# Sparse attention on one core: the inverse row sums are turned in 32 by 32 blocks and brought to the transposed sums by DMA, so that these are transposed once and not twice

## The reference

```python
# 1: attention over 8 global keys and a window of 96, with a slope per head
scores = q @ k.T / 8 + bias;  scores[~keep] = -1e9
a = exp(scores - max);  a = a / (sum(a) + 1e-9);  x = a @ v          # x: (2, 768, 512)
# 2: token mix of rank 32 and a feed-forward part
u = x + (x.T @ U @ V).T;  x = u + relu(u @ w_ch1) @ w_ch2            # 512 -> 2048 -> 512
# 3: gated part
h = relu(x @ w_in);  a, b = split(h);  out = (a * (w_spatial @ norm(b) + b_spatial)) @ w_out
```

## Time and profile before

| | |
|---|---|
| median of three runs | 494.84 us |
| span of the profiled execution, first to last instruction | 493.2 us |
| what lies around the span, against the median | 1.6 us |
| PE busy | 489.0 us (99%) |
| DVE, ACT, POOL busy | 310.2, 222.0, 250.2 us |
| the 24 steps, from `turn(0)` to `hidden(0)` | 9.24 to 92.15 us |
| granted TensorE clock over the span | 1.00 |

### The profile page before, as it was taken

The page is one execution under the profiler, slowest core; times in us unless marked ns, Lnnn a source line. Parts: engine busy times, 40 slices in busy tenths (PEclk is TensorE's granted clock), DMA queues, the critical chain, the costliest instruction groups (busy, mean ns, idle before and its releaser), DMA issues.

```text
span 493.2 us, 7961 instructions
## 1 busy us (share of the span) xinstructions
PE 489.0 (99%) x2804; PEld 409.3 (83%) x2804; DVE 310.2 (63%) x727; ACT 222.0 (45%) x520; POOL 250.2 (51%) x221
## 2 busy tenths in 40 slices
PE   9999999999999999999999999999999999999997
PEld 8788677887888888888888888888888888998986
DVE  5888788421279456564655656557868888878600
ACT  7988889532234633242332322415433356333122
POOL 5997576443346666854566546232885201950000
PEclk9999999999999999999999999999999999999999
DMA  8734501132222322012222020220213000001022
GB/s 236 236 127 111 191 2 45 46 128 86 81 87 89 129 85 71 31 72 85 85 86 78 8 85 3 84 64 2 64 65 115 4 0 1 1 1 43 23 85 108
DMA packets 14697, 36.29 MB, mean 74 GB/s; under 512 B 2496, under 2 KB 2752, under 8 KB 14656
## 3 DMA queue, kind: packets, MB, share of 16 engines
q1 hardware_dynamic: 12640, 32.35, 19.8%
q10 hardware_dynamic: 2016, 3.41, 1.8%
HBM read 32.61 MB, written 3.15 MB: 72 GB/s over the span
## 4 chain that ended last, share of the span: by engine, by line
PE 82%; DVE 6%; POOL 4%; ACT 3%; issue 2%; DVEq 2%; DMA 1%; SPq 0%; ACTq 0%
PE bank L1792 15%; PE bank L1724 9%; PE bank L1644 9%; PE bank L1874 8%; PE bank L1821 8%; PE bank L1814 8%; PE bank L1513 7%; PE bank L1551 4%; PE bank L1569 4%; PE bank L1536 4%; PE bank L1503 1%; POOL sp_op L587 1%; PE bank L1583 1%; DVE newton L1020 1%; DVEq L1008 1%
## 5 line engine op out<-in xcount | busy, mean ns | idle before, releaser
L532 POOL TENSOR_TENSOR w_slot<-stage,w_slot 128x1024 fp32r<-128x1024 f32 x30 | 73.0, 2445 | 65.4 <-ACT w_slot L1249 65.4
L940 DVE TENSOR_TENSOR uT<-bank,uT 128x512 f32<-128x512 f32 x68 | 45.8, 689 | 25.2 <-PE bank L1821 23.2
L1179 ACT ACTIVATE prob<-prob,row_min 128x256 f32<-128x256 f32 (+1 forms) x96 | 45.9, 480 | 6.9 <-DVE row_min L756 6.8
L1792 PE MATMUL bank<-u_op,s_slot 128*128 128x512 f32 x192 | 47.6, 389 | 0.0
L1724 PE MATMUL bank<-hid,w_slot 128*128 128x512 f32 x192 | 46.9, 393 | 0.0
L1644 PE MATMUL bank<-u_split,w_slot 128*128 128x512 f32 x192 | 46.5, 391 | 0.0
L1814 PE MATMUL bank<-hid,w_slot 128*128 128x512 f32 x192 | 46.1, 389 | 0.0
L1821 PE MATMUL bank<-hid,w_slot 128*128 128x512 f32 x192 | 46.1, 389 | 0.0
L978 DVE TENSOR_TENSOR part<-part,bank 128x512 f32<-128x512 f32 x40 | 27.4, 686 | 26.9 <-PE bank L1792 26.5
L1724 PEld LDWEIGHTS bank<-hid,w_slot 128*128 128x128 f32 x192 | 35.7, 188 | 8.2 <-issue 0.9
L1814 PEld LDWEIGHTS bank<-hid,w_slot 128*128 128x128 f32 x192 | 36.0, 188 | 7.5
(11 more groups left out here) (152 smaller groups left out, 963.5 us busy)
## 6 DMA issues: line engine op xcount, KB each, us to landing
stage<-in_w_ch SPq DMA_DIRECT2D x32, 512.0 KB, 3.3
qk_raw<-in_qk SPq DMA_DIRECT2D x23, 256.0 KB, 4.7
v_all<-in_v SPq DMA_DIRECT2D x12, 256.0 KB, 5.2
out_dram<-o_stage ACTq DMA_DIRECT2D x11, 256.0 KB, 2.0
stage<-in_w_spT SPq DMA_DIRECT2D x6, 384.0 KB, 3.1
stage<-in_w_in SPq DMA_DIRECT2D x4, 512.0 KB, 4.2
stage<-in_w_out SPq DMA_DIRECT2D x2, 512.0 KB, 4.0
V_raw<-in_V SPq DMA_DIRECT2D x4, 96.0 KB, 4.6
```

Of the source, the lines that this page charges most:

```text
L532: nc.gpsimd.tensor_tensor(dst[:, LO, :], stage[n % 2][:, 0:w], dst[:, HI, :].bitcast(F32), ALU.subtract).then_inc(w_lo, 1)
L940: vec.tensor_tensor(y, y_bank(e)[:], y, ALU.add).then_inc(y_sum, 1)
L1179: last = sc.activation(prob[r][:, e, 0:w], prob[r][:, e, 0:w], ACT.Exp, bias=row_min[:, k:k + 1], scale=-1.0, accum_out=row_sum[:, q:q + 1])
L1792: last = mm(seven_bank[held][:], lhs, u_op[op][:, m, k, :], start=not more and k == 0 and p == 0, stop=k == 1 and p == 2, skip_group_check ...
```

## The change

`turn_o`, `take_oT` and the old `take_x` go. The inverse sums are now wanted along the row (one number a query), the same on all 64 partitions of a head. So `invert` writes four columns into a 128 by 128 tile of four 32 by 32 blocks a row, DVE turns the blocks, SP stores the four useful partitions to DRAM (2 KB, 16 pieces of 128 bytes) and reads them back on 64 partitions for each head (`store_inverse`, `spread_inverse`). `scale_x` multiplies o transposed in its bank by that and writes uT at once; `turn_x` transposes uT for x_all, which ACT copies (`take_x`). The 1e-9 moves from ACT to DVE. The gather, fold and mixes move one step later, the fourth mix a step earlier. o and the turned x share two banks by turns.

```diff
-            def take_oT(g):
-                ...
+            def invert(g):
+                q = slice(g % 4 * 4, g % 4 * 4 + 4)
+                dve.wait_ge(expd, 2 * g + 2)
+                vec.tensor_scalar(row_one[:, q], row_sum[:, q], 1e-9, None, ALU.add).then_inc(sum_eps, 1)
+                dve.wait_ge(sum_eps, g + 1)
+                if g >= 2:
+                    dve.wait_ge(inv_turned, g - 1)
+                vec.reciprocal(row_inv[g % 2][:, :, 0].rearrange("p (e m) -> p m e", e=2),
+                               row_one[:, q].rearrange("p (m e) -> p m e", e=2)).then_inc(inv_ok, 1)
+            def turn_inverse(g):
+                dve.wait_ge(inv_ok, g + 1)
+                if g >= 3:
+                    dve.wait_ge(inv_out[(g - 3) % 2], 16 * ((g - 3) // 2 + 1))
+                vec.transpose(inv_T[g % 3][:], row_inv[g % 2][:]).then_inc(inv_turned, 1)
+            def scale_x(g):
+                dve.wait_ge(inv_in[g % 3], 32 * (g // 3 + 1))
                 dve.wait_ge(pv_done, g + 1)
+                vec.tensor_tensor(x_tile(g), x_bank(g)[:, 0:256].rearrange("p (c q) -> p c q", c=2),
+                                  inv_rows[g % 3][:], ALU.mult).then_inc(xT_sb, 1)
...
                 for s in range(-2, QUADS + 1):                      # DVE
-                    if s >= 1 and s - 1 not in OT_AMID:
-                        take_oT(s - 1)
                     if 0 <= s < QUADS and s != 2:
                         take_probT(s)
-                    if s >= 1:
-                        take_x(s - 1)
-                    if 0 <= s < QUADS:
-                        invert(s)
+                    if 0 <= s + 1 < QUADS:
+                        invert(s + 1)
+                    if 0 <= s + 1 < QUADS:
+                        turn_inverse(s + 1)
...
                         score_bias(s + 2)
+                    if s >= 1:
+                        scale_x(s - 1)
...
+            def store_inverse(g):                                   # SP
+                sp.wait_ge(inv_turned, g + 1)
+                sp.dma_start(inv_dram[g, :, :].rearrange("k (a q) -> a k q", a=4),
+                             inv_T[g % 3][0:P:32, :, :]).then_inc(inv_out[g % 2], 16)
+            def spread_inverse(g):
+                sp.wait_ge(inv_out[g % 2], 16 * (g // 2 + 1))
+                if g >= 3:
+                    sp.wait_ge(xT_sb, g - 2)
+                for e in range(2):
+                    sp.dma_start(inv_rows[g % 3][e * D:(e + 1) * D, :, :].rearrange("p m q -> p (m q)"),
+                                 inv_dram[g, 2 * e:2 * e + 2, :].rearrange("m q -> (m q)").partition_broadcast(D)
+                                 ).then_inc(inv_in[g % 3], 16)
...
+                for g in range(QUADS):
+                    if g == 11:
+                        load_v(NT)
+                    store_inverse(g)
+                    spread_inverse(g)
+                    if g % 2 == 0 and g // 2 + 4 < TILES:
+                        load_qk(g // 2 + 4)
+                    if g in (1, 3):
+                        load_v((g + 7) // 2)
+                    if g % 2 and g >= 11 and (g + 3) // 2 < TILES:
+                        load_v((g + 3) // 2)
+                    if g == 6:
+                        load_stage(0)
+                        load_stage(1)
...
+            def take_x(g):                                          # ACT
+                act.wait_ge(x_ps, g + 1)
+                ...
+                sc.activation(x_all[:, t % XS, hq * 256:hq * 256 + 256], x_bank(g)[:, 0:256],
+                              ACT.Copy).then_inc(x_half, 1)
...
-                if g:                                               # PE, weigh
-                    pe.wait_ge(oT_sb, g)
+                if g >= 2:
+                    pe.wait_ge(x_half, g - 1)
```

More of the change, by code:

```diff
@@ L672, in _ @@
                         split_early(1, g // 22)
-                    if g >= 17 and g % 2:
-                        split_u((g - 17) // 2)
+                    for j in range(FIRST):
+                        if g == MIX_AT[j] + 2:
+                            split_u(j)
             with pool.Else():
@@ L904, in _ @@
                     sum_u(j)
-                dve.sem_inc(x_half, QUADS)
             def sum_tokens():
@@ L1262, in _ @@
                         split_stage(0)
+                    if s == GATHER:
                         copy_z(0)
-                    if 0 <= s + 1 < QUADS:
-                        add_eps(s + 1)
-                    if s == 14:
+                    if s >= 2:
+                        take_x(s - 2)
+                    if s == GATHER + 1:
                         round_z(0)
@@ L1282, in _ @@
                         split_stage(1)
-                    if s in (16, 18, 20, 22):
-                        round_u((s - 16) // 2)
+                    for j in range(FIRST):
+                        if s == MIX_AT[j] + 1:
+                            round_u(j)
             with act.Else():
@@ L1299, in _ @@
                     round_u(j)
-                for g in range(2 * NT, QUADS - 2):
-                    take_xT(g)
+                for g in range(2 * NT, QUADS):
+                    wide_take_xT(g)
+                act.wait_ge(w_xT, QUADS)
+                act.sem_inc(xT_sb, QUADS)
+                act.sem_inc(x_half, QUADS - 2)
             for f in range(FT):
@@ L1315, in _ @@
                 if f == 0:
-                    take_xT(QUADS - 2, QUADS)
+                    take_x(QUADS - 2)
                 if f == 1:
-                    take_xT(QUADS - 1)
+                    take_x(QUADS - 1)
                 if f == 4:
@@ L1711, in _ @@
                 pe.wait_ge(w_back, 16 * TILES)
-                for g in range(2 * NT, QUADS - 1):
-                    pe.wait_ge(xT_sb, g)
-                    turn_x(g)
+                for g in range(2 * NT, QUADS):
+                    wide_turn_x(g)
                 pe.sem_inc(scored, QUADS)
@@ L1717, in _ @@
                 hidden(0)
+                turn_x(QUADS - 2)
             def contract(f):
```

165 lines of the change are left out of this document (73 added, 92 removed).

## The result

The changed kernel takes 522.29 us, the median of four runs (520.40 to 523.54), against 494.87 us for the kernel before on the same chip. The ratio is 1.0551 (95% interval 1.0527 to 1.0576): slower by 27.4 us, and 13 us over the forecast of 509.3. The direction was right; the size was half of what came, and just outside the range.

The account below looks back on a forecast made before the run. PE bounds the kernel at 3.46 us a plain step, and a loop of 3.66 would replace it. The terms 3.2 + 4.2 + 2.9 + 0.9 - 0.2 = 11.0, with a 3.5 DMA stall 14.5, gave 509.3 us, range 500 to 521.

Parts of the forecast that it names:

- The loop over minima, exponentials, three small instructions and minima: DVE and ACT in one plain step: the new order closes a loop of 3.66 us, against a step of 3.46.
- SP paces: Rival, chance 0.16: SP's waits for stores between tile loads set the groups' pace, 12.5 us in all, time 522.
- faster: Rival, chance 0.08: the loop falls below 3.18 us, PE stays the bound and each step loses `turn_o`, 488.2 us.
- none: Rival, chance 0.04: a loop at its low end gives back in plain steps what the start takes, 494.8 us.
- Start: First groups: nothing has run ahead, so the new order costs its whole latency, 4.2 us by group 4's minima.
- Plain steps: 16 steps with 256 keys, from group 4 on, each 0.20 us longer through the loop: 3.2 us.
- Stage 2: Gather, fold, mixes and their copies in the loop cost 7.1 us in place of 4.2, so 2.9 more.
- It costs nothing in a plain step: `weigh(s)` now waits for `take_x` on ACT; 0.3 us to spare, so no cost in plain steps.
- Last two steps: Steps without scores at the loop's end: `turn(23)` now waits for its exponentials, 0.9 us more.
- DMAs: Store and two reads per inverse, some 4.2 us, hidden within 8.7 except at one place, 3.5 us.
- The stall at `scale_x(7)`: Group 7's store stands behind tile loads and 1 MB of weights: 12.5 us against 8.7, taken as 3.5 of stall.
- DVE's idle time of 0.30 us: Argument for the faster rival: DVE idles 0.30 us before the minima in a plain step of the kernel before.

Follow-up runs that it names:

- e8: Kernel before plus three unused instructions on DVE ahead of the minima (addition, reciprocal, block transpose, behind a wait for the exponentials): 508.61 us.
- e11: e8 without the addition, so the kernel before with only the unused reciprocal and block transpose ahead of the minima: 499.49 us.
- e16: e8 with its addition of a constant made an addition of two tiles of 128 by 4: 508.28 us.
- e3: Changed kernel without the store and reads of the inverse; x multiplied by a constant: 512.98 us.
- e6: Changed kernel without inverse DMAs, copy of x ahead of the probabilities' copy on ACT, DVE's small instructions behind minima and `scale_x`: 500.35 us.
- e5: Changed kernel with the copy of x ahead of the copy of the probabilities on ACT: 522.44 us.
- e14: Changed kernel with the inverse's DMAs made but its reads not awaited by DVE; x multiplied by a constant: 518.83 us.
- e1: Changed kernel with the addition of 1e-9 back on ACT behind each group's exponentials: 525.41 us.
- e4: Changed kernel with the first two weight loads apart, behind groups 7 and 9, not both behind group 6: 522.92 us.
- e9: Changed kernel without the addition of 1e-9; the reciprocal reads the row sums directly: 522.00 us.
- e10: e6 without the addition of 1e-9: 500.12 us.

## Why the prediction was wrong

The loop over minima, exponentials, three small instructions and minima was the right mechanism, and its size undisturbed was right: 3.66 us forecast, 3.67 in e8. Three terms of the sum failed: the addition, which was costed without its waits for POOL; the product with v behind `take_x`, which was put at nothing in a plain step; and the DMAs, which were costed by one stall and without the loads that wait behind stores. What they share is that each was costed as if only it could be late. The stated range of 500 to 521 was also too narrow by the prediction's own chances: *SP paces* at 522 (0.16), faster (0.08) and none (0.04) lie outside and make 0.28, not 2 in 10. By the sum's own steps:

- **Start, 4.2 forecast, 5.8 measured.** e11, the bare loop without the addition, has 3.9. With the addition it is 5.8 in e16, all at the upper clock, and 7.2 in e8, whose granted clock is 0.53 from 16 to 22 us. The changed kernel has both, additions that wait and a granted clock of 0.91 and 0.72 from 8 to 27 us; in it the two weren't separated.
- **Plain steps, 3.2 forecast: the step that failed first.** I wrote that a small instruction costs 0.25 us behind the one it needs, and took that from the distance of two starts in the earlier trace rows. The same rows held the missing term: the second instruction, one element a partition, takes 1.57 us there and 0.22 in the median of its 12. It ends at 372.52, and this one of POOL at 372.51 (kernel before):

```profile
370.66 1.85 POOL L587 TENSOR_TENSOR sp_op<-stage,sp_op 128x768 fp32r<-128x768 f32 x1 [0.18 <-ACT sp_op L1374]
```

In the changed kernel the additions wait 5.9 us for POOL. e8 and e11 differ by the addition alone, 24 x 0.20 = 4.8 us of chain and the waits, and by 9.1 us of time (508.6 - 499.5): 6.3 in the middle and 3.3 at the start.
- **Stage 2, 2.9 forecast, some 2.3 measured in e3.** e11 and e8 can't show it, since they keep the old order: e11 loses 0.2 us in the whole middle, and e8's 6.5 are 16 x 0.21 = 3.4 of loop and 2.8 of additions that wait. In the new order it is there. From the minima of group 14 to those of group 18 e3 loses 3.1 us and e8 0.95, and 0.8 of either is the loop. The causes are two that were forecast: `copy_z` waits for the gather ahead of the exponentials, and the product with v waits 1.28 us for a copy of x behind the first weight's. Part of the 2.3 is the lower clock behind that wait (eight transposes in 1.97 us). e6, with both loops open, loses nothing in these four steps. So this term was about right.
- **"It costs nothing in a plain step": `weigh` behind `take_x`.** I gave it 0.3 us to spare over two steps. Once the loop varies between 3.6 and 4.6 us the slack is gone in single steps. Between 8 and 118 us PE waits 7.9 us for this copy. What it costs by itself isn't shown: e3's middle is 2.5 us above e8's, but 2.2 of that lie in the four steps of stage 2, and e5, which moved the copy forward, won nothing.
- **Last two steps, 0.9 forecast, 3.8 measured.** e8 has 0.0 and e3 3.5, so it is the new path of x and neither the loop nor the DMAs. It begins a step earlier: group 23's minima come 5.29 us after group 22's in e3, 3.67 in e8. `weigh(22)` waits 2.69 us for `take_x`, which stands on ACT behind the last exponentials, 1.13 us of `round_u` and the copy of the probabilities, and then it runs at 1.98 in place of 1.09. The copy of the probabilities isn't what matters: in e5, without it ahead, the wait is 2.21 and the end 4.3. I had only counted the wait of `turn(23)`.
- **DMAs, 3.5 forecast, 9.3 measured.** The stall at `scale_x(7)` was sized well (4.16). Small transfers don't pass large ones here: the store behind 1.5 MB held SP for 5.0 us. Of the prices of one transfer, 1.5 to 1.8 fits the store (1.7 to 1.9 with nothing ahead), and the read takes 2.6. Left out was what follows from SP's waits: it issues v late (some 3.7 of the 5.8 us of e14 over e3), and five more groups wait for their reads, 6.0 us together. *SP paces the groups*, the rival that gave 522, is not what happened, though its number fits, which is luck: there are six waits and not one a group, and without any DMA 18 us remain. It is right in part: SP's waits for stores do delay loads.
- **DVE's idle time of 0.30 us and *Faster*:** it decides at a loop of 3.46. e11 is at that point and is 4.5 us slower, for the start alone.

The terms don't add. Limits stand close behind one another (loop, DMA chain, copy of x, POOL). That fits that the DMAs cost 9.3 us in one setting and 19.0 in another, and that e1, e4, e5 and e9 each took a cause away and won nothing. How the 27.4 us divide is thus known only along one path of kernels: e11 4.6, the addition 9.1, the path of x without DMAs 4.4 (e3 less e8), the DMAs 9.3. Another order of steps would give other shares.

No version here beats the kernel before. e10, with the DMAs left out, comes nearest, and stays at 500; that another order would do better isn't excluded.

## What to carry to other kernels

A loop in which several engines hand work round has as many limits as chains through it. After removing work from the bounding engine, write down the length of every loop over one and over two steps, and the slack of each; where slacks are under half a microsecond, expect a disturbance in one to appear in another, and a forecast that adds single terms to be too low. Before putting a small instruction into such a loop, look at what GpSimd does at that moment: an addition of 128 by 4 cost up to 1.27 us here. A row that looks out of proportion, as the 1.57 us in the earlier trace rows, is the hint. In e8 an addition that changes nothing cost 9.1 us, more than the 6.6 that the change could take from PE. And a queue on which an engine waits for its own stores delays every load written behind it, so price the loads too.

## What was new in the hardware's behaviour

- An addition on DVE from SBUF to SBUF takes 0.14 to 0.16 us alone and up to 1.27 behind an instruction of POOL (mostly a TENSOR_TENSOR, also a cast or a copy), with a constant or with a second tile; reciprocal (0.15 to 0.18) and block transpose (0.31) don't wait.
- A block transpose of 128 by 128 takes 0.31 us, 0.23 from start to start; addition, reciprocal and transpose, each needing the one before, cost 0.63 us together from the first start to the next instruction's (e8), 0.65 forecast.
- After a wait of some 2 us PE's products may take 1.97 us where they take 1.09, or may not: e8 and e16 differ in that behind the same wait of 2.0 us, e14 and e3 behind one of 1.55.
- 2 KB to DRAM, with SP's wait for it, take 1.7 to 1.9 us from issue to the next issue with nothing ahead, up to 3.1 behind a tile's loads and 5.0 behind 1.5 MB. A broadcast to 128 partitions as one read let `scale_x` start 3.8 to 5.3 us after its issue ended; each of two reads of 64 partitions lands 2.6 us after its own.
